# Attention and two feed-forward stages on one core: values ahead of the last turnings, two sums ahead of gates and one copy ahead of a gate

## The reference

```python
mask = q_bucket[:, :, :, None] == k_bucket[:, :, None, :]
scores = np.where(mask, scale * np.matmul(q, k.transpose(0, 1, 3, 2)), -1000000000.0)
attn = softmax(scores)                      # with 1e-09 added to the sum
x = np.matmul(attn, v)                      # 2 batches, 8 heads, 768 positions, 64 columns
...
x = np.maximum(np.maximum(x @ w1, x @ w2), x @ w3) @ w_out      # 1536 x 512, inner 768
...
h = x @ w_in                                # 512 -> 2048
g = h * (1.0 / (1.0 + np.exp(-1.702 * h)))
return g @ w_out2                           # 2048 -> 512
```

## Time and profile before

| | us |
|---|---|
| median of 3 runs | 674.52 |
| lowest and highest | 674.25, 674.67 |
| profiled execution | 674.64 |
| its span, first to last instruction | 672.8 |
| PE busy in the span | 665.3 (99%) |
| DVE, POOL, ACT busy | 492.3, 473.1, 345.4 |
| PE clock granted, mean | 0.999 of full speed |

### The profile page before, as it was taken

One profiled execution on the slowest core, in us unless ns is written; L12 is line 12 of the kernel. 1 busy time (PEld: TensorE's weight loads), 2 busy tenths in 40 slices (PEclk: granted clock), 3 DMA queues, 4 the chain that ended last, 5 costly groups with the idle time before them and its releaser, 6 DMA issues.

```text
span 672.8 us, 11966 instructions
## 1 busy us (share of the span) xinstructions
PE 665.3 (99%) x3892; PEld 577.3 (86%) x3892; DVE 492.3 (73%) x978; ACT 345.4 (51%) x759; POOL 473.1 (70%) x538
## 2 busy tenths in 40 slices
PE   8999999999999999999999999999999999999998
PEld 6776777777777699999999999888989898989896
DVE  6877887788788799869788963668777665555554
ACT  6777777877777630011104453555554555454433
POOL 6774756788886899968860528798887677777710
PEclk9999999999999999999999999999999999999999
DMA  6674836638352111111110201212222224212102
GB/s 138 148 176 110 190 84 157 148 88 190 86 132 81 34 32 32 32 33 33 35 37 25 95 1 35 76 48 81 82 87 64 63 77 143 64 63 64 44 19 94
DMA packets 58492, 54.17 MB, mean 81 GB/s; under 512 B 28640, under 2 KB 47488, under 8 KB 58432
## 3 DMA queue, kind: packets, MB, share of 16 engines
q1 hardware_dynamic: 56784, 53.02, 29.3%
q10 hardware_dynamic: 1648, 0.39, 0.3%
HBM read 32.51 MB, written 3.15 MB: 53 GB/s over the span
## 4 chain that ended last, share of the span: by engine, by line
PE 90%; POOL 6%; issue 1%; DVE 1%; ACT 1%; DVEq 0%; POOLq 0%; ACTq 0%
PE psO L1537 10%; PE psS L1515 9%; PE psR L1523 8%; PE psR L1620 8%; PE psR L1621 8%; PE psR L1622 7%; PE psS L1620 6%; PE psS L1621 6%; PE psS L1622 6%; PE psS L1723 4%; PE psS L1722 4%; PE psS L1721 4%; POOL w_lo L730 2%; PE psR L1463 1%; POOL probs L571 1%
## 5 line engine op out<-in xcount | busy, mean ns | idle before, releaser
L571 POOL TENSOR_SCALAR probs<-probs,lone,inv 128x768 f32<-128x768 f32 x96 | 93.8, 983 | 59.5 <-DVE inv L1136 59.4
L730 POOL TENSOR_TENSOR w_lo<-w_raw,w_hi 128x256 fp32r<-128x256 f32 x96 | 78.8, 833 | 45.7 <-ACT w_hi L974 45.0
L1119 DVE TENSOR_REDUCE neg_max<-psS 128x1 f32<-128x768 f32 x96 | 91.1, 950 | 14.0 <-PE psS L1515 10.3
L797 ACT ACTIVATE probs<-psS,neg_max 128x768 f32<-128x768 f32 x96 | 86.4, 900 | 17.5 <-DVE neg_max L1119 17.3
L554 POOL TENSOR_SCALAR w_hi<-w_raw 128x256 fp32r<-128x256 f32 (+1 forms) x79 | 48.7, 619 | 51.0 <-PE psS L1622 29.6
L806 ACT ACTIVATE probs_t<-psR 128x384 f32<-128x384 f32 x129 | 59.7, 490 | 30.9 <-PE psR L1523 30.5
L1523 PE MATMUL psR<-ident,probs 128*128 128x128 f32 x576 | 74.9, 273 | 0.5 <-POOL probs L571 0.2
L1523 PEld LDWEIGHTS psR<-ident,probs 128*128 128x128 f32 x576 | 66.3, 140 | 6.0 <-POOL probs L571 2.9
L1537 PE MATMUL psO<-probs_t,v_raw 128*64 128x384 f32 x384 | 68.8, 494 | 0.1
L1372 DVE TENSOR_TENSOR v_raw<-psR,early 128x384 f32<-128x384 f32 x64 | 35.3, 552 | 31.4 <-PE psR L1622 31.2
L1377 DVE TENSOR_TENSOR v_raw<-v_raw,bits 128x384 f32<-128x384 f32 x64 | 50.3, 788 | 8.4 <-ACT bits L997 6.0
(11 more groups left out here) (275 smaller groups left out, 1881.6 us busy)
## 6 DMA issues: line engine op xcount, KB each, us to landing
w_raw<-in_moe_w_in SPq DMA_DIRECT2D x16, 512.0 KB, 3.5
w_raw<-in_moe_w_out SPq DMA_DIRECT2D x32, 256.0 KB, 2.7
w_raw<-in_moe_w SPq DMA_DIRECT2D x9, 512.0 KB, 3.8
h_lo<-w_hi SPq DMA_DIRECT2D x22, 192.0 KB, 3.5
h_hi<-w_hi SPq DMA_DIRECT2D x18, 192.0 KB, 3.3
w_raw<-in_q SPq DMA_DIRECT2D x16, 192.0 KB, 3.3
v_raw<-in_v SPq DMA_DIRECT2D x16, 192.0 KB, 2.5
stacks<-w_hi SPq DMA_DIRECT2D x16, 192.0 KB, 3.3
```

The lines of the kernel that those rows point to most:

```text
L571: pool.tensor_scalar(probs[i % PROBS][:, :], probs[i % PROBS][:, :], lone[:, i % 6:i % 6 + 1], inv[:, i % 6:i % 6 + 1], ALU.add, ALU.mult) ...
L730: pool.tensor_tensor(in2_slot(w_lo, n, which), in2_raw(n, PARTS2[which]), f32(in2_slot(w_hi, n, which)), ALU.subtract).then_inc(in2_split, 1)
L797: act.activation(probs[i % PROBS][:, :].rearrange("p (a b) -> p a b", a=2), psS[i % 2][:, :, 0:HALF], ACT.Exp, bias=neg_max[:, i % 6:i % 6 ...
L1119: dve.tensor_reduce(neg_max[:, i % 6:i % 6 + 1], psS[i % 2][:, :, 0:HALF], AX.XY, ALU.min).then_inc(max_ready, 1)
```

## The change

Four edits, all of them changes of order; no instruction is added or taken out.

1. **End of attention, n = 32.** On PE the second half of `times_values` for unit 14 moves ahead of the first nine transposes of the group (tiles 93, and 94's first half). ACT does `x_hi_unit(14)` ahead of its two copies of turned halves. DVE does `x_lo_unit(14)` ahead of `copy_turned(93, 0)`.
2. **ACT, fourth product:** `first_copy(1)` moves ahead of `g_hi(0, 2)` and `sigmoid(0, 3)`.
3. **DVE, fourth product, groups 1 to 15 but not 2:** `mix(n, 5)` moves ahead of `gate(n, 1)`, `mix(n, 6)` ahead of `gate(n, 2)`.
4. **DVE, group 2:** `mix(2, 5)` moves also ahead of `g_lo(2, 0)`, `mix(2, 6)` ahead of `g_lo(2, 1)`.

```diff
--- before.py
+++ after.py
@@ -872,14 +872,16 @@
             exp_tile(11)
             for n in range(4, GROUPS + 1):
                 p, st = n // 4, n % 4
+                if n == GROUPS:
+                    x_hi_unit(n // 2 - 2)
                 copy_turned(3 * n - 3, 1)
                 if n < GROUPS:
                     exp_tile(3 * n)
                 copy_turned(3 * n - 2, 0)
                 if n < GROUPS:
                     exp_tile(3 * n + 1)
-                if n % 2 == 0:
-                    x_hi_unit(n // 2 - 2)
+                    if n % 2 == 0:
+                        x_hi_unit(n // 2 - 2)
                 if st < 2 and p + 1 < PAIRS:
                     for j in range(2):
                         copy_qk(2 * p + 2 + st, j)
@@ -1038,11 +1040,11 @@
             in2_hi(1, 4)
             in2_hi(1, 5)
             in2_hi(1, 6)
+            first_copy(1)
             g_hi(0, 2)
 
 
             sigmoid(0, 3)
-            first_copy(1)
             g_hi(0, 3)
             in2_hi(2, 0)
             out2_hi(2)
@@ -1220,7 +1222,7 @@
                 p, st = n // 4, n % 4
                 if n < GROUPS:
                     row_max(3 * n)
-                copy_turned(3 * n - 3, 0)
+                    copy_turned(3 * n - 3, 0)
                 invert_sums(3 * n - 1, 1)
                 if n < GROUPS:
                     row_max(3 * n + 1)
@@ -1426,12 +1430,19 @@
                 mix(n, 3)
                 gate(n, 0)
                 mix(n, 4)
-                g_lo(n, 0)
+
+                if n != 2:
+                    g_lo(n, 0)
+                mix(n, 5)
+                if n == 2:
+                    g_lo(n, 0)
                 gate(n, 1)
-                mix(n, 5)
+                if n == 2:
+                    mix(n, 6)
                 g_lo(n, 1)
+                if n != 2:
+                    mix(n, 6)
                 gate(n, 2)
-                mix(n, 6)
                 g_lo(n, 2)
                 if n == FPS2:
                     copy_result(0, COPIES[1][0])
@@ -1595,13 +1606,16 @@
                 halves = [(i, j) for i in range(3 * n - 3, 3 * n) for j in range(2)]
                 if n < GROUPS:
                     scores(3 * n)
-                for i, j in halves[:3]:
-                    turn_probs(i, j)
-                if n < GROUPS:
+                    for i, j in halves[:3]:
+                        turn_probs(i, j)
                     scores(3 * n + 1)
                 u, part = (n - 3) // 2, (n - 3) % 2
                 for c in range(TH * part, TH * part + TH):
                     times_values(u, c)
+
+                if n == GROUPS:
+                    for i, j in halves[:3]:
+                        turn_probs(i, j)
                 if st < 2 and p + 1 < PAIRS:
                     turn_qk(2 * p + 2 + st)
                 if st == 2 and p + 1 < PAIRS:
```

## The result

The changed kernel is slower: 675.98 us in the median of 19 runs (675.28 to 676.32), against 674.44 (673.91 to 675.15) for the kernel before (also 19 runs). The ratio is 1.0021, with a 95% interval of 1.0014 to 1.0028: a loss of 0.2%, small but clear of the noise. The forecast was 674.2 us, and its range ended at 675.6. The profiled execution has a span of 674.3 us in place of 672.8.

The account below looks back on a forecast made before the run. PE, busy 665.3 of 672.8 us, was taken as the bound, so reordering could recover only its waits. Terms +0.26 + 0.5 - 0.99 - 0.1 = -0.33 us gave a 674.2 us median, range 673.1 to 675.6.

Parts of the forecast that it names:

- Edit 1, the place itself: End of attention: PE newly waits 0.85 us behind a DVE copy, products begin 0.26 later; bounds -0.58 and +0.4.
- Edit 1, what follows: From attention to the fourth product: nothing found to take up the shift, since other engines wait for PE; no term.
- Edit 2: Group 1, ACT's copy: PE's 0.24 wait goes, but `up2(1, 3)` stands 0.34 to 0.56 later; taken as +0.5 us.
- the ring: Fourth product: ACT, DVE and POOL waiting on each other without slack; said to move 0.42 to 0.64, taken as 0.6 us.
- Edit 4: Group 2: mix 5 fills idle DVE time, PE's waits of 0.78 and 0.21 at group 3 go; -0.99 us.
- Edit 3, groups 1 to 7: Mixes ahead of gates outside group 2: -0.1 us, ends +0.1 and -0.2; a small wait left at `up2(5, 1)`.
- Edit 3, group 8: Covered only by the claim that groups 6 on have no wait now and none then; no term.
- C: Rival, all groups but 2: gates pay, DVE stands bare for ACT's rounding; 675.8, up to 676.5 us; chance 0.13.
- A: Rival, end of attention: the copy holds nobody, -0.58 in place of +0.26; 673.4 us; chance 0.12.
- B: Rival, whole change: A holds and ACT's moved copy does the ring no harm; -1.85, 672.7 us; chance 0.07.
- D: Rival, group 3: the 0.78 wait is POOL's after all, only the 0.21 goes; +0.55, 675.1 us; chance 0.10.
- The four terms that were worked out: Attention +0.26, ACT's copy +0.5, group 2's mixes -0.99, other groups' mixes -0.1; sum -0.33 us.

Follow-up runs that it names:

- e1: Kernel before with only the end-of-attention reorder on PE, ACT and DVE: 675.09 us against 674.42, ratio 1.0010.
- e6: e1 with POOL's first weight sum held until x_lo of unit 14 is made: 674.81 us against 674.15 for the kernel before, ratio 1.0008.
- e2: Kernel before with only ACT's `first_copy(1)` moved ahead of `g_hi(0, 2)` and `sigmoid(0, 3)`: 674.96 us against 674.42, ratio 1.0008.
- e9: Kernel before with the changes of e5 and e7 joined, ACT's first copy left in place: 673.13 us against 674.65, ratio 0.9979.
- e10: Changed kernel with e5's attention order and group 8 ordered as before: 674.16 us against 674.65 for the kernel before, ratio 0.9993.
- e3: Kernel before with only group 2's mixes 5 and 6 moved ahead of remainder and gate: 674.63 us against 674.42, ratio 1.0003.
- e7: Kernel before with only the DVE mix moves, in groups 1 to 7 (group 2 in its own order): 673.70 us against 674.15, ratio 0.9990.
- e4: Changed kernel with group 8 alone in the old order: 675.17 us against 674.42 for the kernel before, ratio 1.0010.
- e5: e1 with DVE's copy that empties psR1 ahead of x_lo of unit 14: 674.48 us against 674.15 for the kernel before, ratio 1.0004.
- e8: e7 with group 4 in the order of group 2: 673.67 us against 674.15 for the kernel before, ratio 0.9991.

## Why the prediction was wrong, step by step

The forecast's sum was -0.33 us; the trace gives +1.36, and with a last score that starts 0.11 later +1.5.

**Edit 1, the place itself: right.** Forecast a wait of 0.85 behind a DVE copy that ends at 228.32, products 0.26 later. Measured 0.85, a copy that ends at 228.42, and 0.22. (The prediction's own figures give 229.42 - 229.15 = 0.27.)

**Edit 1, what follows: the step that failed first.** The prediction said "From there to the fourth product I find nothing that would take up a shift of this size, since the other engines wait for PE there". DVE doesn't wait there: its list runs without idle time for some 27 us, and its pace depends on whose turn it is with POOL. The step only asked whether a shift would be absorbed, never whether it would grow. The prediction put this term at nothing; it measured +0.68 (e1: +0.93 in all; e6: +0.26 with the turns put back).

**Edit 2: right.** Forecast +0.5, with PE 0.34 to 0.56 later at `up2(1, 3)` and the ring 0.6. Measured in e2: +0.52 at `up2(1, 3)`, 0.60 for the ring, and +0.59 at the end; 0.56 between e9 and e10. The mechanism, a ring without slack, is the one described. It was under-sized by 0.1.

**Edit 4: right at its place.** Forecast -0.99, both waits of group 3 gone; they went, with the two instructions behind them that is -1.14, and the reading against the bracket of the earlier trace rows held. But "Next late is nothing in that group" was true of that group alone: by itself the edit gives back all of it in groups 3 and 4 (e3).

**Edit 3, groups 1 to 7: the sum about right, the split wrong.** The forecast booked -0.99 for group 2 and -0.1 for the rest. Of e7's -0.88, nothing comes from group 2 alone (e3: +0.01); the rest is what keeps it. The term itself is +0.21 in the changed kernel, outside its ends of +0.1 and -0.2. `up2(5, 1)` still waits for 0.20 (0.27 forecast), and PE, being early, now also meets `mix(4, 4)` at `up2(4, 6)` (0.14 + 0.08), for which the prediction had no term. It is no different without edit 2: e7 has the same two waits.

**Edit 3, group 8: the second step that failed.** "Groups 6 on have no wait now and none then" was read off PE's waits alone. It needed the slack of every wait of PE in those groups, and one had only 0.75 us: the first `out2` of the second batch, for the results copy on ACT. In this group DVE is ahead of PE, so a sum has to wait for its product, and the new order makes the gate behind it wait as well. The prediction put this term at nothing; it measured +0.65 of waiting and 0.08 behind it, 0.75 in e4.

**The rivals.** The time (675.98) fell in what C, the slower rival, gave: 675.8 to 676.5. Its condition came true, gates that don't wait for POOL (0.62 in group 4, 0.80 and 0.55 in group 8) and a `g_lo` with 0.59 of idle time ahead. Its place didn't: by its sum, without attention, `up2(5, 1)` would have stood 0.99 us later. In the changed kernel it stands 0.64 later with attention's 0.92 in it, that is 0.28 earlier, and the ring isn't longer: POOL's splits are 0.63 late behind edit 2 and 0.69 at group 5. So the time in C's bracket is luck. In group 8 C's mechanism has a share, the 0.59 of idle time ahead of `g_lo(8, 1)`, but the price is set by the results copy. A and B fell with the wait of 0.85 (the copy holds), D with the waits of group 3 (both went).

The four terms that were worked out add up to -0.33 and measured +0.22 + 0.63 - 1.14 + 0.21 = -0.08. Two of them lie a little outside their bounds (edit 2, edit 3). The two that had no term, 0.68 and 0.73, are the miss; 0.03 of the 1.36 have no row.

## What to carry to other kernels

A shift that an edit leaves behind is to be followed along every engine that has no idle time, and not only asked whether someone absorbs it: here two engines that take turns made 0.93 us out of 0.22. When instructions of an engine change places, list the slack of all waits that hang on the ones moved back, above all once-only ones such as the hand-over between batches, since a wait that doesn't show today has a slack of unknown size and no row. And put work that waits for the bottleneck ahead of work that doesn't only where the ring is the late one: the same kind of swap was worth 0.9 us in groups up to 7 and cost 0.75 in group 8.

## What the runs showed of the hardware that I had not expected

- **The order of turns of DVE and POOL sets the speed of both.** A DVE sum of 128x768 took 1.10 to 1.42 us and the next one 1.03 or 1.38, POOL's copy of 128x256 took 1.12 or 0.40. The copy was held (1.11 to 1.12) where the sum began 0.25 us or more ahead of it (before, e5, e6), and not where the two began within 0.03 (e1, the changed kernel). Four kernels give the same relation between the first two sums and the start of x_lo of unit 15 after DVE's last copy of attention: 2.13 and 11.40 (before), 2.23 and 11.50 (e6), 2.45 and 11.73 (e5), 2.62 and 11.89 (after).
- **From the end of a DVE or ACT instruction to the start of the product that waits for it** it is 0.14 to 0.15 us at most waits (228.42 to 228.56, 551.34 to 551.49 in e8, 553.66 to 553.80), and 0.05 at two (242.21 to 242.26, 261.40 to 261.45), though PE stood still there too. Why it is shorter there stays open.
- **The instruction behind a held one starts late as well**, by 0.08 us at the waits of the fourth product (456.63 to 456.88 in place of 0.17) and by 0.11 at 242.26 and 261.45. A wait is worth that much more than its length.
- **The release named in a row's bracket can be wrong** where a product waits for several semaphores: POOL's split in the earlier trace rows and at 433.39, a DVE remainder at 553.80. Each time the true one ended 0.14 to 0.15 ahead of PE.
